# Output gates computed chunk by chunk as (1 + tanh(o/2))/2 within the attention steps, and the first expert weights loaded in half-megabyte pieces over sixteen steps

## The reference

```python
# 1: gated linear attention, a recurrence over tokens t
m_new = np.maximum(f_gate[:, :, t] + m, i_gate[:, :, t])
f_stab = np.exp(f_gate[:, :, t] + m - m_new); i_stab = np.exp(i_gate[:, :, t] - m_new)
C = f_stab * C + i_stab * outer(v_t, k_t);  n = f_stab * n + i_stab * k_t
h_tilde = C @ q_t;  denom = max(|n . q_t|, 1)
o = 1.0 / (1.0 + np.exp(-o_gate[:, :, t]))
y[:, :, t] = o * h_tilde / denom
# x: (3072 tokens, 320) = y of all heads side by side
# 2: soft mixture of 8 experts with 4 slots each: w1 (8, 320, 1024), w2 (8, 1024, 320)
logits = x @ phi
slot_input = softmax(logits, over tokens).T @ x
slot_out[e] = max(slot_input[e] @ w1[e], 0) @ w2[e]
x = softmax(logits, over slots) @ slot_out
# 3: dense MLP, w_in (320, 2048), w_out (2048, 320)
h = x @ w_in;  out = max(h, 0)**2 @ w_out
```

## Time and profile before

| | us |
|---|---|
| median of 3 runs | 419.45 (417.29 to 423.09) |
| the profiled execution | 420.38, of which 418.7 is the span |
| PE busy | 371.7 (89% of the span) |
| DVE busy | 245.1 (59%) |
| ACT busy | 216.2 (52%) |
| POOL busy | 84.4 (20%) |

### The profile page before, as it was taken

The page is one execution under the profiler, slowest core; times in us unless marked ns, Lnnn a source line. Parts: engine busy times, 40 slices in busy tenths (PEclk is TensorE's granted clock), DMA queues, the critical chain, the costliest instruction groups (busy, mean ns, idle before and its releaser), DMA issues.

```text
span 418.7 us, 9229 instructions
## 1 busy us (share of the span) xinstructions
PE 371.7 (89%) x3404; PEld 311.7 (74%) x3404; DVE 245.1 (59%) x569; ACT 216.2 (52%) x381; POOL 84.4 (20%) x102
## 2 busy tenths in 40 slices
PE   0179999879989989689958999999999999999996
PEld 0167777658767767332427999999999999999996
DVE  8426879822795797540164556556556556556553
ACT  5844455333345554303045666656666666566653
POOL 6036656324473663000050000000000000000000
PEclk9999999985699999759995999999999999999999
DMA  7838769997569750999930001001001001001001
GB/s 236 311 81 223 220 198 315 332 238 184 159 218 271 201 157 9 357 363 378 292 111 2 2 1 64 0 2 63 0 0 63 0 0 63 0 0 56 10 0 64
DMA packets 31379, 54.85 MB, mean 131 GB/s; under 512 B 2544, under 2 KB 22704, under 8 KB 31024
## 3 DMA queue, kind: packets, MB, share of 16 engines
q1 hardware_dynamic: 31344, 54.38, 42.0%
HBM read 49.86 MB, written 4.42 MB: 130 GB/s over the span
## 4 chain that ended last, share of the span: by engine, by line
PE 73%; DVE 11%; DMA 9%; SPq 3%; ACT 2%; issue 2%; POOL 0%; DVEq 0%
PE heads_banks L1055 7%; PE heads_banks L1056 7%; PE high_banks L1056 7%; PE high_banks L1055 7%; PE high_banks L1057 7%; PE heads_banks L1057 7%; PE low_banks L1043 5%; PE low_banks L773 5%; PE heads_banks L794 5%; DMA qk_in<-in_qk 4%; PE low_banks L967 3%; DMA wo_raw<-in_w_out 3%; PE high_banks L809 2%; PE heads_banks L787 2%; PE low_banks L825 2%; PE low_banks L762 2%
## 5 line engine op out<-in xcount | busy, mean ns | idle before, releaser
L720 ACT ACTIVATE relu_h<-low_banks 128x512 f32<-128x512 f32 x96 | 57.5, 599 | 67.9 <-PE low_banks L1043 67.6
L1354 DVE CAST sq_hi<-sq_h 128x512 fp32r<-128x512 f32 x96 | 41.0, 427 | 74.6 <-ACT sq_h L725 74.0
L1356 DVE TENSOR_TENSOR sq_lo<-sq_h,sq_hi 128x512 fp32r<-128x512 f32 x96 | 66.5, 693 | 3.3
L725 ACT ACTIVATE sq_h<-relu_h 128x512 f32<-128x512 f32 x96 | 60.7, 632 | 3.0
L1055 PE MATMUL heads_banks<-wo_hi,sq_hi 128*128 128x320 f32 x192 | 60.0, 313 | 1.8 <-DVE sq_lo L1356 1.8
L1056 PE MATMUL heads_banks<-wo_lo,sq_hi 128*128 128x320 f32 x192 | 59.9, 312 | 0.0
L1055 PE MATMUL high_banks<-wo_hi,sq_hi 128*128 128x320 f32 x192 | 59.8, 311 | 0.0
L1056 PE MATMUL high_banks<-wo_lo,sq_hi 128*128 128x320 f32 x192 | 59.8, 311 | 0.0
L1057 PE MATMUL high_banks<-wo_hi,sq_lo 128*128 128x320 f32 x192 | 59.8, 311 | 0.0
L1057 PE MATMUL heads_banks<-wo_hi,sq_lo 128*128 128x320 f32 x192 | 59.6, 310 | 0.0
L1096 DVE TENSOR_TENSOR att_w<-low_banks,att_w 128x512 f32<-128x512 f32 x48 | 30.9, 686 | 34.4 <-PE low_banks L773 21.1
(11 more groups left out here) (163 smaller groups left out, 527.0 us busy)
## 6 DMA issues: line engine op xcount, KB each, us to landing
w_sb<-in_w SPq DMA_DIRECT2D x8, 1280.0 KB, 14.3
w_a<-in_w SPq DMA_DIRECT2D x8, 1024.0 KB, 10.1
qk_in<-in_qk SPq DMA_DIRECT2D x48, 160.0 KB
kv_in<-in_kv SPq DMA_DIRECT2D x24, 320.0 KB, 6.7
fade_b<-fade_scratch SPq DMA_DIRECT2D x40, 80.0 KB
out<-out_sb SPq DMA_DIRECT2D x5, 640.0 KB, 3.2
wo_raw<-in_w_out SPq DMA_DIRECT2D x4, 640.0 KB, 12.7
w_b<-in_w SPq DMA_DIRECT2D x8, 256.0 KB, 11.4
```

The costliest lines, as they stand in the source:

```text
L720: act.activation(relu_h[:, slot], bank[slot][:, :], ACT.Relu).then_inc(relu_done, 1)
L725: act.activation(sq_h[:, slot], relu_h[:, slot], ACT.Square).then_inc(sq_done, 1)
L1354: dve.tensor_copy(sq_hi[:, slot], sq_h[:, slot]).then_inc(hi_done, 1)
L1356: dve.tensor_tensor(sq_lo[:, slot], sq_h[:, slot], sq_hi[:, slot].bitcast(F32), ALU.subtract).then_inc(lo_done, 1)
```

## The change

1. **Gates.** `load_o` is now a load of one chunk (160 KB) into a ring of three buffers `o_in`, issued during step n for step n + 2, and the first two within the prologue. ScalarE computes tanh(o/2) of a chunk in two halves (`half_tanh`) within step n, behind the copy of the heads and ahead of the copy of x. The sigmoids of the prologue are gone, and with them two loads of activation tables: Exp's is loaded first and no other follows. VectorE multiplies (1 + tanh) by the turned heads in one instruction in place of two, and doubles the denominator to make up for the missing factor of a half.
2. **Prologue order.** GpSimd's `log_i` waits for `log_f` and no longer only for `m_run`. ScalarE's exponential of `cum` (`fade`) stands ahead of `keyw` and of the first decays. The stores of `fade`, `cum` and `src`, and the loads of chunk 2, stand earlier in SP's queue.
3. **First expert weights.** `w1` comes in sixteen pieces of 512 KB, one per step from n = 1 to n = 16, and with every second of them a piece of 256 KB.
4. `comb_parts` has a place of its own.

```diff
         def half_of(r, j):
-            def load_o(b):
-                sp.dma_start(gate_o(b), o_gate[b]).then_inc(o_loaded[b], 16)
+            def load_o(b, c):
+                n, s = step(b, c), c % 3
+                at_least(sp, gate_ready, n - 2)
+                sp.dma_start(o_in[:, s], o_gate[b][:, c, :]).then_inc(o_loaded[s], 16)
...
-            for c in loads(0):
-                pass
-            for c in loads(1):
-                load_w1(W1_EARLY[2 * c:2 * c + 2])
-            for c in loads(2):
-                if c > 2:
-                    sp.wait_ge(x_ready, step(2, 0))
-                    load_w1(W1_LATE[2 * (c - 3):2 * (c - 2)])
+            for n in range(STEPS):
...
+                    load_qk(*far)
+                    load_kv(*far)
+                if n + 2 < STEPS:
+                    load_o(*after(*after(b, c)))
+                if 0 <= n - W1_FIRST_STEP < 2 * E:
+                    load_w1_main(*W1_PARTS[n - W1_FIRST_STEP])
+                    if (n - W1_FIRST_STEP) % 2 == 1:
+                        load_w1_rest((n - W1_FIRST_STEP) // 2)
...
-            pool.wait_ge(gate_vec, G_M)
+            pool.wait_ge(gate_vec, G_LOGF)
             pool.tensor_tensor(log_i[:, :], i_in[:, :], m_run[:, 1:1 + S], ALU.subtract)
...
-            def sigmoid(b):
-                act.wait_ge(o_loaded[b], 16)
-                act.activation(gate_o(b), gate_o(b), ACT.Sigmoid).then_inc(sig_ready, 1)
+            def half_tanh(b, c):
+                n, s = step(b, c), c % 3
+                act.wait_ge(o_loaded[s], 16 * (n // 3 + 1))
+                at_least(act, x_ready, n - 1)
+                for odd in range(2):
+                    own = slice(2 * odd, 2 * (odd + 1))
+                    ins = act.activation(gates[:, c % 2, own], paired(o_in[:, s], odd), ACT.Tanh, scale=0.5)
+                ins.then_inc(gate_ready, 1)
...
-                for odd in range(2):
-                    own = slice(2 * odd, 2 * (odd + 1))
-                    ins = dve.tensor_tensor(x_gated[:, own], turned_ps[:, own, :, 0:D], paired(gate_o(b)[:, c], odd), ALU.mult)
-                ins.then_inc(norm_step, 1)
+                dve.scalar_tensor_tensor(out=x_gated, in0=gates[:, c % 2], scalar=1.0, in1=turned_ps[..., 0:D],
+                                         op0=ALU.add, op1=ALU.mult).then_inc(norm_step, 1)
```

More of the change, by code:

```diff
@@ L99, in build_program @@
         slot_acc = sb("slot_acc", [P, KC * P])
+        comb_parts = sb("comb_parts", [P, NC, 4, NS])
         slot_sum = sb("slot_sum", [TS, 1])
@@ L152, in build_program @@
             x_gated = sb("x_gated", [P, HP, 2, D], stack=own)
-            gate_late = sb("gate_late", [P, 2, NC, DM], stack=own)
+            o_in = sb("o_in", [P, 3, DM], stack=own)
+            gates = sb("gates", [P, 2, HP, 2, D], stack=own)
             xT = sb("xT", [P, KC, TRI, L], stack=own)
@@ L178, in build_program @@
             row_rcp = sb("row_rcp", [P, NC], stack=own)
-            comb_parts = sb("comb_parts", [P, NC, 4, NS], stack=own)
         with ExitStack() as own:
@@ L214, in build_program @@
         kv_loaded = [sem(f"kv_loaded{i}") for i in range(3)]
-        o_loaded = [sem(f"o_loaded{i}") for i in range(B)]
+        o_loaded = [sem(f"o_loaded{i}") for i in range(3)]
         rows_loaded = [sem(f"rows_loaded{i}") for i in range(ROW_RING)]
@@ L302, in build_program @@
         G_START, G_M, G_FM, G_LOGF, G_CUM, G_SRC, G_CUMLO, G_SRCLO, G_KEYW = range(1, 10)
-        A_CUM, A_SRC, A_KEYW, A_FADE = range(1, 5)
+        A_CUM, A_SRC, A_FADE, A_KEYW = range(1, 5)
         decay_bank, score_bank = bank[0:2], bank[2:4]
@@ L316, in build_program @@
         head_rows_in = att_w[0:QUAD + H, 1, 0:HP]
-        W1_EARLY = [(e, "a") for e in range(6)] + [(e, "b") for e in range(4, E)]
-        W1_LATE = [(e, "a") for e in range(6, E)] + [(e, "b") for e in range(4)]
+        W1_FIRST_STEP = 1
+        W1_PARTS = [(e, k) for e in range(E) for k in range(2)]
         def half_of(r, j):
@@ L383, in load_src, with load_w1_main, load_w1_rest @@
                     sp.dma_start(row_y[QUAD * r:QUAD * r + H, b % 2].bitcast(F32), rows).then_inc(src_loaded[b % 2], 16)
[L385 to L393, removed]
+            def load_w1_main(e, k):
+                sp.dma_start(w1_a[:, e, k], w1[e, P * k:P * (k + 1), :]).then_inc(w1_loaded, 16)
+            def load_w1_rest(e):
+                p0 = DP * (e % 2)
+                sp.dma_start(w1_b[p0:p0 + DM_LAST, e // 2], w1[e, 2 * P:DM, :]).then_inc(w1_loaded, 16)
             sp.wait_ge(cleared, 1)
@@ L402, in _ @@
             load_kv(0, 1)
+            load_o(0, 0)
             def direct_cum(k):
@@ L431, in _ @@
             sp.dma_start(src_dram, src_parts[:, :, :].bitcast(F32)).then_inc(rows_stored, 16)
+            load_qk(0, 2)
+            load_kv(0, 2)
+            load_o(0, 1)
+            sp.wait_ge(cleared, 3)
+            sp.dma_start(phi_sb[:, 0:2], phi[0:2 * P, :].rearrange("(k p) s -> p k s", p=P)).then_inc(phi_loaded, 16)
+            sp.dma_start(phi_sb[0:DM_LAST, 2], phi[2 * P:DM, :]).then_inc(phi_loaded, 16)
             sp.wait_ge(rows_stored, 48)
@@ L440, in _ @@
             sp.wait_ge(rows_direct, 128)
[L442 to L455, removed]
-            for c in loads(0):
-                pass
-            for c in loads(1):
-                load_w1(W1_EARLY[2 * c:2 * c + 2])
-            for c in loads(2):
-                if c > 2:
-                    sp.wait_ge(x_ready, step(2, 0))
-                    load_w1(W1_LATE[2 * (c - 3):2 * (c - 2)])
-            for c in loads(3, last=True):
-                pass
+            for n in range(STEPS):
+                b, c = n // NC, n % NC
+                if c == 1 and b + 1 < B:
+                    load_src(b + 1)
+                if n + 3 < STEPS:
+                    far = after(*after(*after(b, c)))
+                    if step(*far) >= ROW_RING:
+                        load_rows(*far)
+                    if far[1] > 0 and far != (0, 3):
+                        load_fades(*far)
+                    load_qk(*far)
[6 more added lines that the diff above has]
+                        load_w1_rest((n - W1_FIRST_STEP) // 2)
             def load_w2(experts):
@@ L646, in _ @@
             copy_v(0, 0)
-            for b in range(1, B):
-                sigmoid(b)
-            act.preload_act_table(ACT.Exp)
+            act.activation(fade[:, :], cum[:, :], ACT.Exp).then_inc(gate_act, 1)
             act.wait_ge(gate_vec, G_KEYW)
@@ L652, in _ @@
             decays(0, 0)
-            act.activation(fade[:, :], cum[:, :], ACT.Exp).then_inc(gate_act, 1)
             def act_step(b, c, half, nxt=True, cur=True, prev=True, rb=None):
@@ L661, in act_step @@
                     copy_heads(b, c)
+                    half_tanh(b, c)
                 if prev:
```

28 lines of the change are left out of this document (9 added, 19 removed).

## The result

The changed kernel takes **433.1 us** (median of 4 runs, 427.8 to 433.8) where the kernel before took 418.8 beside it: a ratio of 1.030, with a 95% interval of 1.018 to 1.041. It is slower, outside the forecast's 400 to 415 us. The profiled execution took 433.84 us, of which the span is 432.0; that of before was 418.7, so 13.3 us are to be explained.

What follows compares the result with a forecast made beforehand. It took TensorE as the bound in undisturbed steps, with short urgent transfers delayed in two DMA queues, in the prologue and behind w1. 420.38 - 4.1 (prologue) - 11.4 (w1) = 404.9, predicted 405 us, range 400 to 415.

Steps and rivals of the forecast that it cites:

- Do they?: Attention steps: asked whether all waits on loads go once w1 is spread; judged yes, with 311 GB/s to be had.
- need of 283 GB/s: Sixteen attention steps: load rate required, 1.61 MB per undisturbed step of 5.68 us.
- rival C: Attention steps: DMA engines don't keep up, 237 GB/s at full share, 6.8 us a step; 413 us, chance 0.10.
- the lead of two steps: Attention steps: loads issued ahead give late data two steps' time, about 10 us, absorbing the first part of a shortfall.
- the 11.4 us: Attention steps: waits and low-clock matmuls from w1's present placing, 38.46 against 27.06 us; taken as gained in full.
- D: Attention steps: late loads also drop TensorE to 1.2 GHz, three 11.4 us events in place of one; 439 us, chance 0.07.
- The prologue: Before the steps: gates leave the queue, `row_y` lands sooner, first decay matmul near 18.3 us; gain 4.1 us.
- rival B: Prologue's gain does not pass on, since first steps wait for something else such as the fades; 409 us, chance 0.11.
- Gates in the steps: ScalarE's tanh, 338 ns per half and 0.68 us a step, fits into its idle waits: cost 0 us.
- sum of 1573 KB: Attention steps: bytes loaded per step, covering q, k, v, fades, 160 of gates and 512 + 128 of w1.
- `log_i`: Prologue: running it after `log_f` speeds that up but meets the scan `cum` on the shared SBUF port; gain 0.
- The tail: After the attention's last scores, w2, w_in and w_out loads: not shortened, passes earlier gains to the end in full.

Runs made afterwards that it cites:

- e6: Changed kernel with the last rows of w1 loaded for two experts at once, four 512 KB loads on 128 partitions replacing eight of 256 KB on 64: 422.7 us, ratio 1.022.
- e7: Changed kernel with each 512 KB piece of w1 loaded as two DMAs onto 64 partitions each, same bytes: 451.6 us, ratio 1.091.
- e2: Kernel before with only w1 spread, one 512 KB piece a step and 256 KB every second step; gates and prologue as before: 424.4 us, ratio 1.012.
- e5: Changed kernel with all of w1 loaded after the loads of the last step: 434.4 us, ratio 1.048.
- e12: Kernel before, sigmoids still in the prologue, with w1 in twenty 512 KB pieces, one per step: 413.6 us, ratio 0.985.
- e3: Changed kernel with the load of `phi` back ahead of the stores of the fades: 428.0 us, ratio 1.020.
- e10: e9 with w1's twenty 512 KB pieces one to a step, steps 1 to 20, so no step carries two: 412.7 us, ratio 0.981.
- e1: Changed kernel with w1 placed as in the kernel before; gates per chunk and new prologue stay: 426.1 us, ratio 1.016.
- e9: Changed kernel with both e3's place of `phi` and e6's load of w1 on 128 partitions: 418.2 us, ratio 1.000.
- e11: e10 with the gates of three chunks in one load of 480 KB: 410.8 us, ratio 0.980.

## Why the prediction was wrong

**The step that failed** is the one headed "Do they?": "With the queue full and a mixture of the same loads the trace shows 297, 349 and 288, a mean of 311, so 0.91 of what can be had." The need of 283 GB/s was compared with a supply that this mixture doesn't have. In the change's own full windows it was 246 and 228, and 262 at full share over the middle of the steps. The three windows of the earlier trace rows held mostly 1 MB pieces of w1 on 128 partitions. The 64-partition pieces were issued at 78.16 and 88.12 and landed 9.3 us or more later, so they fall into the third window in part and into the fourth, at 204 GB/s and a share of 0.86. The 237 at full share that the fourth gives was in hand, as rival C. Averaging the three and giving the fourth one chance in ten was the mistake. e6 and e7 show what sets it: full windows move 286 or 184 GB/s by the number of loads on half the partitions. Why the same eight half-partition pieces cost more when spread than when bunched, as e2 against before has it (1.2%; 266 against 290 GB/s), is not settled. That the kernel before issues them in pairs, one for each half, is hardly the reason, for e7's come in such pairs too.

**What followed** was rival C's cause at a price above C's. C had 237 GB/s, and full windows showed 246 and 228. It priced that at 18 us over sixteen steps, let the lead of two steps absorb 10, and still took the 11.4 us as gained. Instead GpSimd waited for k and v 15 times, 60.5 us in all, and the steps took 13.7 us more than before: no part of the 11.4 came, and the lead did not absorb the rest. The clock fell again and again, as D said, but each time for less long. D's threefold cost isn't there, since the mean is 0.93 against 0.92 before. D's 439 us lies near the 433.8 of the profiled run, by luck in part. What of the 13.7 us each wait and each stretch of low clock cost is not taken apart by any run.

**The term of 11.4 us** for what the present placing of w1 costs is borne out: e5 gives 11.9, on another chip and if gates in the steps cost nothing. Taking it in full was wrong: the change turned 11.9 into 25.6. e12, with a better stream, gained 5.7 of it in the steps (130.1 against 135.8, by profiles from different chips).

**The prologue.** `row_y` landed as forecast: the first decay matmul starts at 17.91 (forecast 18.3), 4.5 us sooner than before. That this passes on failed at the second decay, which waited 5.04 us for `phi`. The diff moves that load behind three stores and chunk 2's loads, and the forecast didn't follow it past them. With `phi` back (e3), the first score starts 4.5 us sooner than before. But e10 and e12 show that even then the end does not: the steps with the gates in them give it back. That is rival B's outcome, by another way than B's.

**Gates in the steps.** The tanh takes 327 ns (forecast 338), and e5's steps run at full clock with it, so as far as shown it hides, as said. What the forecast counted only inside its sum of 1573 KB is that the gates' loads left a stretch with room to spare. e1 puts 1.6% on gates and prologue order together, all of it in the steps (142.5 us against 135.8); how it divides between the loads and ScalarE's work is not shown.

**`log_i`** came out as worked out. Chain of after:

```profile
7.57 3.05 POOL log_i L531
10.64 0.95 DVE src L1256
```

`src` starts at 10.64; before it was 10.62. `log_f`, now without `log_i` beside it, takes 0.94 us instead of 2.19. The scan took 1.74 us and GpSimd's subtraction beside it 3.05 instead of 2.30, near the 1.74 + 1.39 that the forecast gave the two one after the other. That they take turns is as the Trainium skill (SBUF — State Buffer, Who interferes with whom) has it: nothing gained, nothing lost.

**The tail** passed on what it got (254.8 against 254.2), still fed by `wo_raw`, which landed 44.7 us after the last score.

## What to carry to other kernels

Spreading a large load over more steps helped here only where the stream of all loads at full share exceeded the need of 283 GB/s: at 262 the kernel lost 3%, at 296 it was level (e9), and at 294 with no step carrying two pieces it gained 2% (e10). Read that rate from windows with the same mixture of shapes, and let the worst window decide, not the mean. Weigh each load by the partitions that it reaches, and repack loads for 64 partitions into half as many for 128 before touching their order. A microsecond gained ahead of a stage counts only if that stage does not give it back: compare the start of its last piece of work, not of its first. And follow every DMA that a diff moves, with its first reader, past everything that it now stands behind.

## What the runs showed of the hardware

- The same bytes in loads for 64 partitions instead of 128 took a full window from 286 to 184 GB/s, the engines' time from 178.8 to 206.4 us, and the kernel from 422.7 to 451.6 us (e6 and e7).
- Loads for 40 rows made into loads for 48, 20% more bytes in them, cost 2 to 3% and took a fifth more of the DMA engines' time. The Trainium skill (DMA: Bandwidth & Descriptors, Why a DMA increments its semaphore by 16 and not by 1) has 40 rows on 10 DMA engines and, by the same rule, 48 on 16; more engines per load, if they were used, did not help here.
- Half-megabyte pieces on 128 partitions, one to a step, cost nothing that shows: with them e12 was 1.5% faster than the kernel with 1 MB pieces, the repacked 256 KB ones included. The Trainium skill (DMA: Bandwidth & Descriptors, Bandwidth) advises 1 MiB or more; here what the load reaches and when it comes decided.
- TensorE's granted clock had a mean of 0.93 in the middle of the change's steps, 0.91 in the kernel before, and 1.00 in e5 and e11 with the same matmuls, though TensorE waited in e11 too (13.5 us from first to last score).
